# Scores of three head pairs moved from the attention prologue into the first dense chunk, with low halves a step later, one multiply per pair and a query load issued by ScalarE

## What is computed

```python
scores = scale * np.matmul(q, k.transpose(0, 1, 3, 2))
mask = (rel >= 0) & (rel < window)                 # rel = query position - key position
scores = np.where(mask, scores, -1000000000.0)
attn = np.exp(scores - np.max(scores, axis=-1, keepdims=True))
attn = attn / (np.sum(attn, axis=-1, keepdims=True) + 1e-09)
x = np.matmul(attn, v)                             # as (1152, 512)
p = domain_probs / (domain_probs.sum(-1, keepdims=True) + 1e-09)
for e in range(4):                                 # dense mixture
    out += p[:, e:e + 1] * (np.maximum(x @ w1[e], 0.0) @ w2[e])
...
for e in range(8):                                 # routed mixture, tokens with skip score > 0
    y[mask] = gate_w[mask, None] * (np.maximum(xc[mask] @ u1[e], 0.0) @ u2[e])
```

## Time and profile before

| what | us |
|---|---|
| median of three runs | 649.08 |
| lowest, highest | 648.16, 649.21 |
| the profiled execution, its own time | 648.53 |
| its span, first to last instruction | 646.9 |
| PE busy | 622.0 |
| DVE busy | 297.4 |
| ACT busy | 246.6 |
| POOL busy | 76.3 |

### The profile page before, as it was taken

How to read it: one execution, slowest core, us unless ns; L and a number is a source line. 1 busy time by engine, 2 the same in 40 slices (tenths; PEclk the granted TensorE clock), 3 DMA queues, 4 the chain that set the end, 5 groups by cost and what they waited for, 6 DMA issues and landing times.

```text
span 646.9 us, 9656 instructions
## 1 busy us (share of the span) xinstructions
PE 622.0 (96%) x3410; PEld 555.7 (86%) x3411; DVE 297.4 (46%) x784; ACT 246.6 (38%) x518; POOL 76.3 (12%) x119
## 2 busy tenths in 40 slices
PE   5799999999999999999999999999999999999994
PEld 4688989898989898989899998989888888888883
DVE  5765566634412124512124424445567644771770
ACT  4764445522401013301113321312334754862871
POOL 6560000000000000000000001000012321221221
PEclk9899999999999999999999999999999999999998
DMA  8912232304999996310002221042346967692640
GB/s 262 264 54 86 62 97 91 124 1 150 223 262 232 254 241 198 92 61 0 0 0 70 106 100 60 13 136 75 97 158 209 358 216 248 211 360 54 199 129 9
DMA packets 51232, 89.98 MB, mean 139 GB/s; under 512 B 13112, under 2 KB 17720, under 8 KB 51200
## 3 DMA queue, kind: packets, MB, share of 16 engines
q1 hardware_dynamic: 47760, 82.30, 42.8%
q0 software_dynamic: 3440, 7.26, 4.5%
HBM read 63.88 MB, written 27.08 MB: 141 GB/s over the span
## 4 chain that ended last, share of the span: by engine, by line
PE 90%; DMA 2%; ACT 2%; DVE 2%; issue 1%; SPq 1%; POOL 1%; DVEq 0%; POOLq 0%; ACTq 0%
PE ps_y L999 31%; PE ps_h L999 29%; PE ps_y L1073 9%; PE ps_h L1073 9%; PE ps_o L958 2%; PE ps_s L933 2%; PE ps_s L1088 2%; PE ps_s L978 1%; PE ps_t L946 1%; DMA raw<-u 1%; PE ps_o L1053 1%; DMA raw<-w 1%; PE ps_h L1021 1%; PE ps_t L1062 1%; ACT prob L580 1%
## 5 line engine op out<-in xcount | busy, mean ns | idle before, releaser
L626 ACT ACTIVATE ht_hi<-ps_h 128x384 fp32r<-128x384 f32 (+1 forms) x104 | 48.6, 467 | 240.0 <-PE ps_h L999 231.2
L999 PE MATMUL ps_h<-xt_hi,w_hi_a 128*128 128x384 f32 (+1 forms) x400 | 131.1, 328 | 1.2 <-DVE ht_lo L814 1.2
L999 PE MATMUL ps_h<-xt_hi,w_lo_a 128*128 128x384 f32 (+1 forms) x400 | 129.4, 324 | 0.0
L999 PE MATMUL ps_h<-xt_lo,w_hi_a 128*128 128x384 f32 (+1 forms) x400 | 129.4, 323 | 0.0
L999 PE MATMUL ps_y<-w_hi_a,ht_hi 128*128 128x512 f32 x288 | 115.5, 401 | 0.3 <-POOL w_lo_a L451 0.3
L999 PE MATMUL ps_y<-w_hi_a,ht_lo 128*128 128x512 f32 x288 | 112.7, 391 | 0.0
L999 PE MATMUL ps_y<-w_lo_a,ht_hi 128*128 128x512 f32 x288 | 112.4, 390 | 0.0
L814 DVE SCALAR_TENSOR_TENSOR ht_lo<-ps_h,ht_hi 128x384 fp32r<-128x384 f32 (+1 forms) x104 | 54.8, 526 | 118.5 <-ACT ht_hi L626 118.1
L999 PEld LDWEIGHTS ps_h<-xt_hi,w_hi_a 128*128 128x128 f32 x400 | 75.4, 188 | 2.1 <-DVE ht_lo L814 1.8
L999 PEld LDWEIGHTS ps_h<-xt_lo,w_hi_a 128*128 128x128 f32 x400 | 75.4, 188 | 0.4
L999 PEld LDWEIGHTS ps_h<-xt_hi,w_lo_a 128*128 128x128 f32 x400 | 75.3, 188 | 0.0
(11 more groups left out here) (149 smaller groups left out, 836.2 us busy)
## 6 DMA issues: line engine op xcount, KB each, us to landing
raw<-u SPq DMA_DIRECT2D x40, 512.0 KB, 4.6
x_sorted<-xg SPq DMA_DIRECT2D x4, 4112.0 KB, 44.7
raw<-w SPq DMA_DIRECT2D x32, 512.0 KB, 4.6
x<-u SPq DMA_DIRECT2D x24, 512.0 KB, 5.8
vt<-v SPq DMA_DIRECT2D x17, 256.0 KB, 2.9
xg<-x_sorted POOLq DMA_DIRECT2D x12, 257.0 KB
kt<-k SPq DMA_DIRECT2D x8, 384.0 KB, 4.8
x_sorted<-xg SPq DMA_DIRECT2D x1, 2313.0 KB, 43.5
```

Of the source, the lines that this page charges most:

```text
L626: a.activation(ht_hi[:, pos, 0:P * tiles], ps_h[:, pos % 2, 0:P * tiles], ACT.Relu).then_inc(h_hi_done, 1)
L999: ins = mm(dst, hi_lo[l], rhs_hi_lo[r], start=(first and n == 0), stop=(last and n == 2))
```

## The change

It has four parts. The scores, mask and exponential of pairs 8, 9 and 10 leave the prologue and become `("scores", p)` entries of chunk 0's table; with them the table has eleven steps at positions 0, 2, 4, ... 20. The normalisation of pairs 8 and 9 and the transpose and copy of pair 8 go with them (in the steps of scores 9 and 10). In the prologue, DVE makes the low halves a step later, except at its last step. For pairs 0 to 7 DVE's normalisation writes the reciprocal to PSUM (a spare bank, ps_h) and multiplies both halves of a pair in one operation. The keys of tile 0 are loaded first, and one of the two query loads of tile 0 is issued by ACT.

```diff
         if c < len(FIRST_CHUNKS) - 1:
             begin, end = (steps_for(sum(FIRST_CHUNKS[i])) for i in (c, c + 1))
             room = FC + FIRST_CHUNKS[c][1] * FC - 1
-            for n, p in enumerate(range(begin, end)):
-                at.setdefault(n * room // (end - begin), []).append(("attention", p))
+            steps = [("attention", p) for p in range(begin, end)]
+            if c == 0:
+                steps = [("scores", p) for p in range(begin - LAG - 1, begin)] + steps
+            for n, step in enumerate(steps):
+                at.setdefault(n * room // len(steps), []).append(step)
...
+        def load_queries(engine, t, j):
...
-            load_keys(0)
+            sp.dma_start(kt[:, 0, :, WINDOW:KEYS],
+                         k[:, 0:P].rearrange("(a p) n -> p a n", p=P)).then_inc(keys_landed[0], 16)
+            load_queries(sp, 0, 0)
             load_values(0)
...
+            load_queries(act, 0, 1)
             for p in range(PROLOGUE):
                 attention(p)
...
+            def normalise(r):
+                dve.wait_ge(probs_ready, 2 * r + 2)
+                b = 2 * r % BUFFERS
+                if r < EARLY:
+                    inverse = ps_h[:, 1, b:b + 2]
+                    link(d.tensor_scalar(inverse, sums[:, b:b + 2], EPS, None, ALU.add))
+                    link(d.reciprocal(inverse, inverse))
+                    d.tensor_tensor(prob[:, b:b + 2, :], prob[:, b:b + 2, :],
+                                    inverse.unsqueeze(2).broadcast_to([P, 2, P]), ALU.mult).then_inc(probs_normal, 2)
+                else:
...
+            def scores(p):
+                mask_scores(p)
+                if p > EARLY:
+                    normalise(p - 1)
...
+                if p < EARLY or PROLOGUE <= p < NPAIR:
+                    mask_scores(p)
+                r = p - 1
+                if 0 <= r < EARLY or PROLOGUE - 1 <= r < NPAIR:
+                    normalise(r)
+                if p < PROLOGUE - 1:
+                    r = p - LAG - 2
+                else:
+                    r = p - LAG - 1
```

More of the change, by code:

```diff
@@ L288, in build_block @@
         block = ctx.enter_context(nc.Block())
+        def load_queries(engine, t, j):
+            own = slice(HD * j, HD * j + HD)
+            engine.dma_start(qz[own, t % 3, :, :, j, :].rearrange("p a s n -> p (a s) n"),
+                             q[own, t].rearrange("p a (s n) -> p (a s) n", s=HALVES)).then_inc(keys_landed[t % 3], 16)
         @block.sync
@@ L319, in load_keys @@
                 for j in range(2):
-                    own = slice(HD * j, HD * j + HD)
-                    sp.dma_start(qz[own, b, :, :, j, :].rearrange("p a s n -> p (a s) n"),
-                                 q[own, t].rearrange("p a (s n) -> p (a s) n", s=HALVES)).then_inc(keys_landed[b], 16)
+                    load_queries(sp, t, j)
                 lo = max(0, n0 - WINDOW)
@@ L573, in weights_hi, with copy_probs @@
                 copy(dst, ring[:, j, :]).then_inc(done, 1)
-            def attention(p):
[L576 to L581, removed]
-                r = p - LAG
[L583 to L588, removed]
+            def scores(p):
+                for u in (2 * p, 2 * p + 1):
+                    act.wait_ge(scores_masked, u + 1)
+                    own = prob[:, u % BUFFERS, :]
+                    a.activation(own, own, ACT.Exp, bias=least[:, u % BUFFERS:u % BUFFERS + 1], scale=-1.0,
+                                 accum_out=sums[:, u % BUFFERS:u % BUFFERS + 1]).then_inc(probs_ready, 1)
+                if p == PROLOGUE - 1:
+                    copy_probs(EARLY)
+            def copy_probs(r):
+                act.wait_ge(pt_ready, r + 1)
+                if r >= 2:
+                    act.wait_ge(pv_done, r - 1)
+                copy(prob_t[:, r % 2].rearrange("p s n -> p (s n)"), ps_t[:, 0:HALVES * P]).then_inc(pt_copied, 1)
+            def attention(p):
+                if p < EARLY or PROLOGUE <= p < NPAIR:
+                    scores(p)
+                r = p - LAG
+                if 0 <= r < EARLY or PROLOGUE - LAG <= r < NPAIR:
+                    copy_probs(r)
                 r -= 1
@@ L611, in beside @@
                         attention(*what[1:])
+                    elif what[0] == "scores":
+                        scores(*what[1:])
                     elif what[0] == "first_weights":
@@ L723, in weights_lo, with mask_scores @@
                 minus_hi(lo, ring[:, j, :], hi).then_inc(split, 1)
[L725 to L740, removed]
+            def mask_scores(p):
+                dve.wait_ge(scores_ready, p + 1)
+                if p >= LAG + 2:
+                    dve.wait_ge(pt_ready, p - LAG - 1)
+                for half in range(HALVES):
+                    u = 2 * p + half
+                    m = (p // PAIRS * HALVES + half) % (SEQ // WINDOW) == 0
+                    d.tensor_tensor_reduce(out=prob[:, u % BUFFERS, :], in0=ps_s[:, p % 2, P * half:P * half + P],
+                                           in1=mask[:, int(m), :], scale=SCALE, scalar=3e38, op0=ALU.add, op1=ALU.min,
+                                           accum_out=least[:, u % BUFFERS:u % BUFFERS + 1]).then_inc(scores_masked, 1)
+            def normalise(r):
[8 more added lines that the diff above has]
+                else:
                     link(d.tensor_scalar(sums[:, b:b + 2], sums[:, b:b + 2], EPS, None, ALU.add))
@@ L745, in attention, with scores @@
                                         ALU.mult).then_inc(probs_normal, 1)
-                r = p - LAG - 1
+            def scores(p):
+                mask_scores(p)
+                if p > EARLY:
+                    normalise(p - 1)
+            def attention(p):
+                if p < EARLY or PROLOGUE <= p < NPAIR:
+                    mask_scores(p)
[6 more added lines that the diff above has]
+                    r = p - LAG - 1
                 if 0 <= r < NPAIR and r % 2:
@@ new lines, in scores @@
+            def scores(p):
+                t, a = p // PAIRS, p % PAIRS
+                if a == 0:
+                    pe.wait_ge(keys_landed[t % 3], 16 * 3 * (t // 3 + 1))
+                if p == PAIRS:
+                    pe.wait_ge(zeroed_more, 4)
+                if p >= 2:
+                    pe.wait_ge(scores_masked, 2 * p - 2)
+                for half in range(HALVES):
+                    last = mm(ps_s[:, p % 2, P * half:P * half + P],
+                              qz[:, t % 3, a, half].rearrange("p j n -> p (j n)"),
+                              kt[:, t % 3, a, WINDOW * half:WINDOW * half + P], start=True, stop=True)
+                last.then_inc(scores_ready, 1)
+                if p == PROLOGUE - 1:
+                    turn_probs(EARLY)
@@ new lines, in turn_probs @@
+            def turn_probs(r):
+                if r == 0:
+                    pe.wait_ge(masks_made, 2)
+                pe.wait_ge(probs_normal, 2 * r + 2)
+                if r >= 1:
+                    pe.wait_ge(pt_copied, r)
+                for half in range(HALVES):
+                    last = turn(ps_t[:, P * half:P * half + P], prob[:, (2 * r + half) % BUFFERS, :], ident[:])
+                last.then_inc(pt_ready, 1)
+            def attention(p):
+                if p < EARLY or PROLOGUE <= p < NPAIR:
+                    scores(p)
+                r = p - LAG
+                if 0 <= r < EARLY or PROLOGUE - LAG <= r < NPAIR:
+                    turn_probs(r)
```

## The result

The changed kernel took 651.4 us as a median of seven runs (649.76 to 652.63). The kernel before had 648.4 in its seven (647.76 to 649.23); the 649.08 that the forecast starts from was the median of its first three. The ratio is 1.0041, with a 95% interval from 1.0026 to 1.0055: about 2.7 us slower, where 0.2 faster, in effect no difference, was forecast, with a range up to 650.6. The profiled execution of the changed kernel took 652.5 and lies near the top of its seven; its span is 650.9, 4.0 above that of before, so its trace shows the loss somewhat larger than the median.

The account below looks back on a forecast made before the run. TensorE, busy 96%, was taken as the bound, with gains only before 48.2 us. Terms 3.4 - 2.24 - 1.0 gave 0.2 us faster, 648.9, in effect no difference; own range 648.4 to 650.4, with rivals 647.1 to 650.6.

Parts of the forecast that it names:

- From the third block to the outputs: Third hidden block to first output matmul: same PE work as before, so 12.0 us kept and outputs start at 44.8.
- The drop: Rival: TensorE's clock falls after PE's idle time before the third hidden block; 1.7 lost, 650.6, 1.5 slower; chance 0.2.
- Scores of pairs 8 to 10 out of the prologue: Prologue's end: dense part starts near 26.5, probs_e lands at 30.7, third hidden block starts at 32.8, 3.4 earlier.
- The gate: Before the third hidden block: DVE needs the late-loaded probs_e before its first low half, and PE waits for that.
- the combinations: Joint outcomes of forecast and rivals, left outside the range 647.1 to 650.6; about 2 in 10.
- First loads: Kernel start: SP issues two loads before the values, not three; 0.7 earlier at the w1 piece gating ACT, bounds 0 and 0.8.
- One multiply: Prologue's eight pairs: one 128x256 multiply replaces two, taken as 0.44, bounds 0.44 and 1.19; no separate gain counted.
- Low halves: Prologue: pair 7's mask no longer waits, gaining 1.3; last w1 low half ends at 25.8, 2.0 earlier; bounds 0.7 and 2.7.
- What is left behind it: Chunk 0's output part: seven attention steps left instead of five, 2.24 given back.
- closer spacing: Chunk 0's output part: steps every two positions make three output products late by 0.33 each, 1.0 given back.
- The faster one: Rival: whole front gain reaches the last w1 low half, probs_e lands at 29.5; 2.0 faster, 647.1; chance 0.25.
- The loads hold everything: Rival: probs_e comes at most 1.9 earlier; 1.3 slower, 650.4; its chance lies within the forecast's 0.55.

Follow-up runs that it names:

- the filled hole: Changed kernel plus 22 unused matmuls of 512 columns on PE ahead of the third hidden block, probs_e still late: 649.56 us, ratio 1.0011.
- the gate open: Changed kernel with the probs_e load issued right after the keys of tile 2, ahead of the last two w2 pieces: 644.84 us, ratio 0.993.

## Why the prediction was wrong

**The steps that failed** are two. In the profile their shares are read from the start of the outputs: 49.33 for a forecast of 44.8, 4.5 later.

The first is "*From the third block to the outputs*", "I leave 12.0", with nothing in it for the clock. It measured 13.9, and 11.3 with the clock held by the filled hole. In the medians this is the larger part: about 1.9, give or take 1.2, of the 2.9 by which the forecast was missed (2.7 slower for 0.2 faster). The drop stood in the text as a rival with 0.2 and 1.5 slower, and its mechanism, its place and nearly its price were right (2.6 in the profile for 1.7). What was wrong is that it was kept out of the forecast: the forecast itself put a hole of 3 us on PE, and a drop had followed a sparser stretch in the trace of before. That a hole of 3 us would have been enough no run shows; those of 5.09 in the changed kernel and 4.06 with only the scores moved were.

The second is the landing of probs_e in "*Scores of pairs 8 to 10 out of the prologue*": "I take 30.7, nearer the lower end, because the queue had gaps there", with 30.2 and 32.2 as bounds. The gate had been named and its place in the sum was right. In the profiled execution it was issued at 28.04 for 27.1 and landed 6.00 later, at 34.04, beyond both bounds; the division behind it was 0.7 shorter than before (1.41 for 2.07 from landing to block), and so the third block came at 35.45 for 32.8. The size came from a queue with gaps, and here the share was over 1.0 from 26 to 34 (0.81 before). An earlier prologue does not always meet a fuller queue: with the same loads in the same order it landed at 31.5 and 31.3 in two other profiles, within the bounds. The share while it was in flight was 1.05 here, 0.61 before and 0.81 to 0.95 in the other four, which fits a fuller queue but does not show it for the cause. Why it was 6.00 in this execution stays open, as does how much of the median's loss this term makes.

The range left out "the combinations", and the result is such a combination: with a late probs_e the hole is longer, and the clock falls in it.

**Point by point.** First loads: 0.7 forecast at the first w1 piece; it landed 0.3 later in this profile (12.54). One profile can't show this term: the first high half of w1 started between 11.0 and 13.5 in nine profiles with the new order, five of them by 11.5, and between 12.3 and 13.6 in five with the old one, three of them by 12.6. Undoing the part cost 0.1%, within the noise. One multiply: 0.42 measured for 0.44 taken. "I count none apart" was not tested behind the gate; with the gate open, the kernel without this part is 3.1 slower. Low halves: right in the mechanism (masks of pairs 5 and 7 behind their scores), 2.9 when undone with the gate open. The last low half of w1 ended at 26.6 for 25.8: it was to gain 2.0, of which 0.7 from the loads, and gained 1.15, with the w1 piece 1.0 later than forecast. First hidden matmul 26.82 for 26.5: right. Third block 35.45 for 32.8, and 13.9 for 12.0 from there to the outputs: wrong, as said. What is left behind it (2.24) and closer spacing (3 x 0.33; measured 3 x 0.35): right to 0.1. In the run with the filled hole, where probs_e landed at 31.5 and the clock stood, outputs start at 44.93 for a forecast of 44.8; that is luck in part, for the third block came 0.8 late (33.61 for 32.8) and the stretch behind it was 0.7 shorter than the 12.0 taken.

**The rivals.** The faster one (the front gives all it can, 647.1) did not come; what an open gate gives is more than it had, 644.2 to 644.8. "The loads hold everything" was right in that probs_e came hardly earlier (34.04 for 34.13), but not in its reason: the last low half of w1 did end 1.15 earlier.

The Trainium skill, TensorE: Matmul & The Clock Gate, section HAM oscillation, says that waits between bursts make the next burst cold. The trace agrees (0.50 from 36 to 40 behind the hole).

## What to carry to other kernels

Before an engine is brought earlier to a stage, list every wait between its arrival and that stage's steady work, the small ones of other engines in their program order included. Here a division whose result is first read more than 20 us later (34.06 and 60.4 us) cost 1.3 us while all came late, and 7 once they came early; move such a wait to its first user first. And where a forecast itself leaves TensorE idle for some microseconds ahead of dense work, its likeliest case has the blocks behind the hole at the lower clock, as behind both holes of 4 to 5 us here.

## What had not been expected of the hardware

The landing of a load of 18 KB behind nearly the same sequence of transfers lay between 3.1 and 6.0 us after its issue in six profiles, and the first high half of w1 started between 11.0 and 13.5 with one and the same order of loads ahead of it. A single profile does not fix such a time; the bounds of a term that rests on it have to be wider than the two ends that one trace gives.

Matmuls without any use, 22 of 512 columns in 5.01 us, made the kernel 0.30% faster: with them the clock did not fall.

Prologues that look alike did not fare alike: with probs_e early and the scores moved, the granted clock was 1.00 from 10 to 48 us with all parts or without the new loads, and 0.50 from 28 to 32 without the new multiply, without the later low halves, or with none of the three. What decides between them no run shows.

One DVE multiply of 128x128 from SBUF took 0.28 with POOL idle (two in a row 0.48) and up to 0.80 beside POOL's subtraction, while the multiply of 128x256 with its second operand in PSUM took 0.42 all eight times, at 8.49 with little on POOL and at 14.90 beside the subtraction.
